# Dense matmuls ahead of each attention chunk, and half of the score mask moved to ScalarE and GpSimd

## What is computed

```python
def _attn_ref(q, k, v, f_logit):
    f = 1.0 / (1.0 + np.exp(-f_logit))
    for t in range(S):
        state = f[:, :, t, :, None] * state + np.einsum('bhd,bhe->bhde', k[:, :, t], v[:, :, t])
        y[:, :, t] = np.einsum('bhd,bhde->bhe', q[:, :, t], state)

def _moe_ref(x, w_in, w_out):          # 384 -> 2048 -> 384
    h = x @ w_in
    return (h * np.tanh(softplus(h))) @ w_out

def _moe2_ref(x, w_gate, w_val, w_out):  # 384 -> 1536 -> 384
    return (sigmoid(x @ w_gate) * (x @ w_val)) @ w_out
```

## Time and profile before

| | |
|---|---|
| median of 3 runs | 1080.47 us (1075.73 to 1088.42) |
| the profiled execution, its own time | 1090.29 us |
| its span, first to last instruction | 1088.4 us |
| TensorE busy, share of the span | 97% |
| VectorE | 49% |
| ScalarE | 43% |
| GpSimd | 12% |
| attention stage, until the first feed-forward matmul | about 220 us |
| the rest | about 869 us |

### The profile page before, as it was taken

One profiled execution on the slowest core, in us unless ns is written; L12 is line 12 of the kernel. 1 busy time (PEld: TensorE's weight loads), 2 busy tenths in 40 slices (PEclk: granted clock), 3 DMA queues, 4 the chain that ended last, 5 costly groups with the idle time before them and its releaser, 6 DMA issues.

```text
span 1088.4 us, 14722 instructions
## 1 busy us (share of the span) xinstructions
PE 1051.7 (97%) x5237; PEld 880.6 (81%) x5237; DVE 536.3 (49%) x770; ACT 464.1 (43%) x777; POOL 134.3 (12%) x146
## 2 busy tenths in 40 slices
PE   5999999989999999999999989999999999999997
PEld 4999988868888788887888878888888888888885
DVE  8576688356666666667777742222222222222221
ACT  2222222157777777777777731122222221321122
POOL 2221222150000000001454450000000000000000
PEclk9999986589999999999999999999999999999999
DMA  5343344110000000000111110000000000100001
GB/s 161 94 122 97 109 144 123 45 58 1 1 1 1 0 0 0 0 0 15 44 47 51 49 37 1 1 1 1 35 24 0 0 0 0 58 1 1 1 1 58
DMA packets 35339, 37.55 MB, mean 35 GB/s; under 512 B 4064, under 2 KB 26080, under 8 KB 35296
## 3 DMA queue, kind: packets, MB, share of 16 engines
q1 hardware_dynamic: 35296, 36.98, 11.4%
HBM read 32.24 MB, written 4.72 MB: 34 GB/s over the span
## 4 chain that ended last, share of the span: by engine, by line
PE 93%; DVE 3%; ACT 2%; issue 1%; DMA 0%; SPq 0%; DVEq 0%; ACTq 0%
PE banks L851 26%; PE banks L853 25%; PE banks L852 25%; PE banks L784 6%; PE banks L766 3%; PE banks L791 3%; PE banks L771 2%; PE banks L801 2%; PE banks L810 1%; DVE suffix L572 1%; DVE prefix L589 0%; DVE xlo L724 0%; DVE glo L716 0%; ACT sets L468 0%; ACT xhi L498 0%
## 5 line engine op out<-in xcount | busy, mean ns | idle before, releaser
L851 PE MATMUL banks<-xhi,whi 128*128 (+1 forms) x720 | 285.5, 396 | 4.1 <-DVE xlo L724 2.6
L853 PE MATMUL banks<-xhi,wlo 128*128 (+1 forms) x720 | 284.0, 394 | 0.0
L852 PE MATMUL banks<-xlo,whi 128*128 (+1 forms) x720 | 281.5, 391 | 0.0
L851 PE MATMUL banks<-ghi,whi 128*128 128x512 f32 x504 | 200.4, 398 | 7.8 <-DVE glo L716 7.5
L853 PE MATMUL banks<-ghi,wlo 128*128 128x512 f32 x504 | 198.5, 394 | 0.0
L852 PE MATMUL banks<-glo,whi 128*128 128x512 f32 x504 | 197.3, 391 | 0.0
L744 DVE TENSOR_TENSOR prod<-prod,banks 128x512 f32<-128x512 f32 x72 | 49.5, 688 | 290.3 <-PE banks L853 290.3
L851 PEld LDWEIGHTS banks<-xhi,whi 128*128 128x128 f32 x720 | 135.9, 189 | 33.7 <-DVE xlo L724 3.0
L853 PEld LDWEIGHTS banks<-xhi,wlo 128*128 128x128 f32 x720 | 135.6, 188 | 32.1
L852 PEld LDWEIGHTS banks<-xlo,whi 128*128 128x128 f32 x720 | 135.9, 189 | 30.8
L517 ACT ACTIVATE prod<-banks 128x512 f32<-128x512 f32 x72 | 43.1, 598 | 188.1 <-PE banks L853 188.1
(11 more groups left out here) (66 smaller groups left out, 1012.6 us busy)
## 6 DMA issues: line engine op xcount, KB each, us to landing
raw<-w_out_dram SPq DMA_DIRECT2D x28, 192.0 KB, 2.4
xb<-f_dram SPq DMA_DIRECT2D x48, 96.0 KB, 2.4
kb<-k_dram SPq DMA_DIRECT2D x48, 96.0 KB, 2.2
qb<-q_dram SPq DMA_DIRECT2D x48, 96.0 KB, 2.2
vb<-v_dram SPq DMA_DIRECT2D x24, 192.0 KB, 2.4
out_dram<-rows_out SPq DMA_DIRECT2D x18, 256.0 KB, 2.1
raw<-w_in_dram SPq DMA_DIRECT2D x16, 192.0 KB, 2.8
raw<-w_gate_dram SPq DMA_DIRECT2D x12, 192.0 KB, 2.4
```

Of the source, the lines that this page charges most:

```text
L851: pe.matmul(ps, hi, xh, start=first, stop=False)
L852: pe.matmul(ps, hi, xl, start=False, stop=False)
L853: return pe.matmul(ps, lo, xh, start=False, stop=last)
```

## The change

Three things, all in the attention stage.

1. `keep_clock` on TensorE: ahead of the scores in steps 4 to 23, four matmuls of 128x128 weights by 384 columns, from the split weights that already lie in SBUF, into a part of PSUM bank 7 that nobody reads.
2. The mask is divided. VectorE masks the even heads' scores alone (128x512 in place of 128x1024). ScalarE copies the odd heads' scores to `probs` unmasked (`odd_scores`), and GpSimd zeroes the upper triangle in place (`mask_odd`, an `affine_select` over 128x512).
3. Semaphores and order with it. TensorE's values wait for VectorE's mask and for GpSimd's (`odd_done`); the next scores wait for ScalarE's copy as well (`copied_done`). GpSimd's step is now the high part of unit t, the wait for the copy of chunk t-1, the low part of unit t, the mask of chunk t-1.

```diff
         def masks_and_weights(b, n):
+                unit, chunk = lag_a(b, n, 0), lag_a(b, n, 1)
+                if unit:
+                    high_unit(*unit)
+                if chunk:
+                    pool.wait_ge(copied_done, chunk[0] * NCH + chunk[1] + 1)
+                if unit:
+                    low_unit(*unit)
+                if chunk:
+                    mask_odd(*chunk)
...
+            def mask_odd(b, n):
+                odd = probs[:, n % 2, PAIRS:H]
+                pool.affine_select(out=odd, in_=odd, compare_op=ALU.is_ge, fill=0.0, base=0,
+                                   pattern=[[0, PAIRS], [1, C]], channel_multiplier=-1).then_inc(odd_done, 1)
...
-            run_a(pool, 0, 0, split_unit)
+            run_a(pool, 1, 1, masks_and_weights)
...
+            def odd_scores(b, n):
+                g = b * NCH + n
+                wait(act, y_done, g - 1)
+                act.wait_ge(scores_done, g + 1)
+                act.activation(probs[:, n % 2, PAIRS:H], s_ps[:, PAIRS:H, :], ACT.Copy).then_inc(copied_done, 1)
...
-                for lag, do in ((0, gates), (1, keep_total), (4, x_high), (2, k_rows), (3, y_rows)):
+                for lag, do in ((0, gates), (1, keep_total), (4, x_high), (2, k_rows), (3, y_rows), (1, odd_scores)):
...
-                dve.tensor_tensor(probs[:, n % 2], s_ps, causal[:, :].unsqueeze(1).to_broadcast([P, H, C]), ALU.mult).then_inc(probs_done, 1)
+                dve.tensor_tensor(probs[:, n % 2, 0:PAIRS], s_ps[:, 0:PAIRS, :], causal[:, :].unsqueeze(1).to_broadcast([P, PAIRS, C]), ALU.mult).then_inc(probs_done, 1)
...
+                wait(pe, copied_done, g)
...
+                pe.wait_ge(odd_done, g + 1)
...
+            def keep_clock():
+                for c in range(KC):
+                    pe.matmul(idle_ps, whi[:, 0, c * P:(c + 1) * P], whi[:, 0, :], start=True, stop=True)
+                pe.matmul(idle_ps, wlo[:, 0, 0:P], whi[:, 0, :], start=True, stop=True)
...
+                if not isinstance(b, int) or B * NCH > b * NCH + n >= 4:
+                    if isinstance(b, int) and (b, n) == (0, 4):
+                        pe.wait_ge(w_ready, 1)
+                    keep_clock()
```

More of the change, by code:

```diff
@@ L168, in attention_mlp_mlp @@
         guard_ps = bank[7][0:1, 0:P]
+        idle_ps = bank[7][:, 0:DM]
         vrow_ps = bank[0][:, :].rearrange("p (a t) -> p a t", a=PAIRS)
@@ L182, in attention_mlp_mlp @@
         total_done, attention_over = sem("total_done"), sem("attention_over")
-        scores_done, probs_done = sem("scores_done"), sem("probs_done")
+        scores_done, copied_done, probs_done, odd_done = sem("scores_done"), sem("copied_done"), sem("probs_done"), sem("odd_done")
         kt_done, ktsb_done = sem("kt_done"), sem("ktsb_done")
@@ L369, in split, with high_unit, low_unit, masks_and_weights @@
                 pool.tensor_tensor(lo, raw[:, s, :], hi.bitcast(F32), ALU.subtract).then_inc(w_ready, 1)
-            def split_unit(b, n):
+            def high_unit(b, n):
+                unit, s = b * NCH + n, n % STAGES
+                pool.wait_ge(raw_in[s], (b * (NCH // STAGES) + n // STAGES + 1) * 16)
+                pool.tensor_copy(whi[:, bass.ds(unit, 1), :].squeeze(1), raw[:, s, :]).then_inc(w_hi_done, 1)
+            def low_unit(b, n):
                 unit, s = b * NCH + n, n % STAGES
                 hi, lo = whi[:, bass.ds(unit, 1), :].squeeze(1), wlo[:, bass.ds(unit, 1), :].squeeze(1)
-                pool.wait_ge(raw_in[s], (b * (NCH // STAGES) + n // STAGES + 1) * 16)
-                pool.tensor_copy(hi, raw[:, s, :]).then_inc(w_hi_done, 1)
                 pool.wait_ge(w_hi_done, unit + 1)
                 pool.tensor_tensor(lo, raw[:, s, :], hi.bitcast(F32), ALU.subtract).then_inc(w_ready, 1)
-            run_a(pool, 0, 0, split_unit)
+            def mask_odd(b, n):
+                odd = probs[:, n % 2, PAIRS:H]
+                pool.affine_select(out=odd, in_=odd, compare_op=ALU.is_ge, fill=0.0, base=0,
+                                   pattern=[[0, PAIRS], [1, C]], channel_multiplier=-1).then_inc(odd_done, 1)
+            def masks_and_weights(b, n):
+                unit, chunk = lag_a(b, n, 0), lag_a(b, n, 1)
[8 more added lines that the diff above has]
+            run_a(pool, 1, 1, masks_and_weights)
             pool.wait_ge(attention_over, 1)
```

## The result

| | before | after |
|---|---|---|
| median | 1084.45 us (1075.73 to 1094.93, 4 runs) | 1189.80 us (1181.83 to 1190.51, 4 runs) |
| ratio | | 1.098, 95% interval 1.089 to 1.108 |
| span of the profiled execution | 1088.4 us | 1188.4 us |
| first feed-forward matmul | 219.7 us | 321.9 us |

A forecast was written before the change was run, and what follows sets the result against it. The prediction took TensorE at its low clock to bound the attention stage. Terms 86.2 + 3.3 + 1.3 - 8 = +83 us on 1090.3 gave 1173, stated as 1172 us; range 1125 to 1194.

The forecast's parts named there:

- The loop: Attention stage: TensorE's values wait for GpSimd's mask, behind the split of a late-loaded weight unit; +86.2 us over 21 steps.
- P: Time from the start of TensorE's attention step until GpSimd's mask lets the values start; 6.6 us (5.5 to 7.6).
- rival C: Attention stage: VectorE's scans and GpSimd's mask obstruct each other, P 7.8 us, +25 us, 1198 us; chance 0.09.
- What follows the wait: TensorE's values and state product after waiting for the mask, at low clock: 123.8 us over 21 steps.
- The high clock's gift: TensorE's clock rises in many attention steps but mostly covers the wait; -8 us (0 to -28).
- Step 2: Early attention step of TensorE: its values wait for the split of unit 1 and the mask; +3.3 us.
- Dense matmuls in step 24: TensorE's dense matmuls in an attention step where nothing hides them; +1.3 us.
- Their cover: Dense matmuls in steps 4 to 23 are hidden under P and cost nothing; uncovered, 26 us.
- A: Attention stage: GpSimd's loop exists but TensorE's high clock holds; 1123 us, chance 0.13.
- B: Attention stage: no loop, GpSimd's mask is in time and TensorE runs at high clock; 1036 us, chance 0.04.

The follow-up runs named there:

- Cut at the split: Changed kernel with GpSimd's split of the weight unit moved one step later, all else kept: 1084.7 us (1036.9 to 1117.0).
- cut at the load: Changed kernel with the weight unit loaded ahead of v in SP's step, GpSimd's order kept: 1122.7 us (1113.8 to 1129.0).
- the memset run: Changed kernel with GpSimd's select replaced by a memset of the same 128x512 tile, odd heads' scores zero: 1171.3 us, ratio 1.078.

## Why the prediction was right, and where it was off

**The loop** was the forecast's mechanism, and each of its links is in the trace of the changed kernel. Cut at the split the loss goes (1084.7 us), cut at the load most of it does (1122.7). The range, 1125 to 1194, held the time with 4 us to spare; the forecast was 18 us short of the measured median, since nearly all errors lay on one side.

**P** was put at 6.6 us and was 7.03 on average. Its terms: 0.72 to the issue (0.77 forecast), 2.98 until the cast (2.8), 1.87 for the split (2.0), 1.26 for the select (0.9), which starts 0.05 us before the recorded end of the subtraction, and 0.26 until the values (0.1). The select was mis-sized, for the reason that was given to rival C: undisturbed it took 0.64 us, less than forecast, but in 14 of 21 steps it met a scan. Rival C's price, a whole scan more, was too high: it lost 0.92 us each time, not 1.2, and not each time. But its mechanism took part: 14 x 0.92 is 12.9 us, and 1189.8 us lies nearer to C's 1198 than to the forecast's 1172. From the select's end to the values it takes 0.26 us, not the 0.1 for which the prediction gave no row. Together 147.6 us where 138.6 stood: +9.0.

The Trainium skill (SBUF — State Buffer, section "Who interferes with whom") has a refinement with which the memset run agrees: a VectorE instruction with two SBUF inputs is in the way of a GpSimd instruction that reads SBUF, and not of one that only writes it. 1.56 us for the select behind a scan, 0.52 for each memset.

**What follows the wait** was put at 123.8 us by the rows of a stream that doesn't stop; behind a wait it was 126.9, as the first group takes 3.55 us to the next and not 3.41. +3.1.

**The high clock's gift** of 8 us never came. The step that failed was "I expect rises in many steps": in the profiled execution none of 21 was seen. Why not one came stays open. With four dense matmuls the clock was high in four of 21 groups in the memset run, and in 13 with the split later; with eight in the loop it rose in most steps. The other half of the argument, that a wait of 1.7 us or more lets high clock cover only a little of the values, fared better: with eight dense matmuls all eight waits of 2.44 us and more were followed by a fall within the step. But behind four of them the values still ran at high clock, and waits alone don't explain the falls. In the kernel with the later split the clock fell where nothing waited at all (its TensorE timeline):

```profile
121.03 1.88 PE L815 MATMUL banks<-vb,probs 128*128 128x48 f32 x16
...
123.87 0.67 PE L832 MATMUL banks<-vb,kt_sb 128*64 128x48 f32 x16
124.47 1.09 PE L847 MATMUL banks<-whi 128*128 128x384 f32 x3
125.36 0.52 PE L848 MATMUL banks<-whi,wlo 128*128 128x384 f32 x1
```

The Trainium skill (TensorE: Matmul & The Clock Gate, section "HAM oscillation — how this bites in real kernels") explains falls by long idle gaps. The falls at the long waits of the run with eight dense matmuls agree with it, and the clock that stayed high behind seven of the eight waits of up to 1.29 us does too. The fall shown here does not: TensorE had no gap ahead of it. The page's section "A second HAM failure mode: psum-queue depth-cycling" puts falls down to short idle between groups; none is seen here either. The traces say more: in the kernel before, a stream of small matmuls without a gap ran at 1.2 GHz for 119 us, from 19.3 to 138.4 us.

**Step 2** came out at +3.9 us (3.3 forecast). **Dense matmuls in step 24**, +1.3 us, was a slip: they stand in steps 4 to 23, as the section on the change says, and all are hidden. The stretch from step 24 on took 19.8 us before and after. **Their cover** held: taking them out gained nothing.

These make the difference on the span: 9.0 + 3.1 + 8.0 + 0.6 - 1.3 = 19.4 us, and -2.2 us in the feed-forward layers. With the forecast's +82.8 us that makes +100.0, which is what the spans say.

**The rivals.** A (high clock holds in the loop, 1123 us) is excluded by 21 groups of 3.6 us; the run with eight dense matmuls lies half way to it, at 1157, and lost the clock within the step at each wait of 2.44 us and more. B (no loop, 1036 us) had its price nearly right: a single execution with the split later took 1036.9 us, at a mean granted clock of 0.988 (its trace wasn't kept).

## What to carry to other kernels

Before an idle engine is given work that another engine waits for, look at what stands ahead of it in its queue, and at what that waits for in its turn. A queue that idles 6 us a step for a transfer is not free; whoever comes to read its result inherits the wait. When only the order is wrong, moving the late item by a step can be enough: here it took the loss of 10% away. The gain of 3.5% came only with six dense matmuls in place of four. And price an operation on GpSimd beside a VectorE scan by the pair, not by the undisturbed row.

## What the runs showed of the hardware

- TensorE stayed at its low level for 119 us in a stream without a gap (kernel before, 19.3 to 138.4 us). The profile's clock row said 1.00 for it, and only the durations gave it away: 3.48 us against 1.88 for the same 16 records.
- With eight dense matmuls in the loop, high clock lasted to the end of the step behind seven of eight waits of 0.44 to 1.29 us, until some way behind the values after four of 2.44 to 3.10 us, and hardly or not at all into the values after four of 3.59 to 3.83 us.
- Extra matmuls that nobody reads were worth their time when there were enough of them. Six of 384 columns a step, ahead of the scores and with the split later, cost 1.25 us at high clock (6.60 against 5.35 us a step), while a step at low clock without any takes 9.87 us. Four in the same place left it to chance (1037 to 1117 us).
- At the low level four dense matmuls of 384 columns delayed the scores by 1.58 us, not the 1.3 us that 512-column ones had led me to expect.
- A 128x512 select on GpSimd takes 0.64 us, or 1.56 if a suffix scan of VectorE began up to 0.89 us before it; a memset of the same tile took 0.52 us in all 24 cases, 15 of them behind such a scan.
